# Three of the six tiles of a Fourier transform made from the other three by a product with a reversing permutation

## The chip, the cores and the metric

The kernel runs on 1 core of one Trainium2 chip. A core has TensorE (PE: matrix products; PEld is its weight load), VectorE (DVE), ScalarE (ACT), GpSimd (POOL) and SyncE (SP, which here issues all DMAs). The metric is the device time of one execution in microseconds, of which the profile's span covers all but 2 us. Lower is better.

## The reference

Three stages follow each other on 4 batches of 768 tokens. The first is an attention with a decaying state, in 8 heads of width 48; its result is x, [4, 768, 384]. The second mixes x by a Fourier transform and a normalised channel product, the third by a product over tokens and one over channels:

```python
def _moe_ref(x, w_ch1, w_ch2):
    X = np.fft.fft(x, axis=1)
    X = np.fft.fft(X, axis=2)
    mixed = np.real(X).astype(np.float32)
    u = x + mixed
    ...
    ch = np.maximum(un @ w_ch1, 0.0) @ w_ch2
    return (u + ch).astype(np.float32)

def _moe2_ref(x, w_tok1, w_tok2, w_ch1, w_ch2):
    xt = x.transpose(0, 2, 1)
    h = np.maximum(xt @ w_tok1, 0.0) @ w_tok2
    u = x + h.transpose(0, 2, 1)
    h2 = np.maximum(u @ w_ch1, 0.0) @ w_ch2
    return (u + h2).astype(np.float32)
```

## The kernel before

The attention runs in 24 chunks of 128 tokens, m = 0 to 23; b = m // 6 is the batch and j = m % 6 the chunk in it. In a chunk TensorE turns keys, makes the scores of chunk m and the output y of chunk m - 1 between them, updates the state, and turns y of chunk m - 1. ScalarE and VectorE do the elementwise work on gates, queries and keys for a part of three chunks, six chunks ahead, in steps that hang on each other: on ScalarE squares, magnitudes (Ln and Exp), inverses, factors, arctangents, sines; on VectorE logs (with a scan), tangents, phases (with a scan), products. Two loads of function tables fall into each part (L776 and L779). The last such part starts with m = 21, so from m = 20 on ScalarE has only copies.

The Fourier transform of batch b - 1 is done between the chunks of batch b. It is called a pass here: pass one is m = 6 to 11, pass two m = 12 to 17, pass three m = 18 to 23; the fourth batch is transformed after the attention. VectorE folds the sequence (fold_sequence), so that 384 rows stand for 768. At j=1 width_transform gives a_sb, cosine part and sine part of 193 columns each (FH = 193, since the other 191 columns mirror them). Then sequence_transform makes six tiles of 128 rows: for each one matmul with alt for the middle row, three with the cosine table cs and three with the sine table ss, all fp32, into the two halves of a bank of PSUM (f_bank, in turn). transformed_at says at which j: tile 0 at 2, tiles 1 and 2 at 3, tiles 3 and 4 at 4, tile 5 at 5. add_transform on VectorE adds a tile to y in four operations (cosines minus sines into the low columns, cosines plus sines mirrored into the high ones); added_at says when, one chunk later at the latest. SyncE stores the rows as u.

The order of the work is written out by hand, one program for each engine, with semaphores between them. An engine does its list strictly in order. In the profile's names h_area holds y_sb, cs and ss, res_area holds a_sb, cd and sd, bank is a bank of PSUM, late_area holds a_mid and small constants, tok_raw holds alt.

After the attention comes the channel product s0. TensorE does the width transforms, the transposes of the first normed batch (L243), six tiles of the sequence transform, then hidden (three fp32r matmuls for each of three k, L233 to L235, 12 tiles). From the third tile on, hidden waits until low_hidden (L209) on VectorE has freed the bank of the tile two before. Between its four-operation adds VectorE makes w2l (low_w2_sixth, L134, six parts) from w2h, which ScalarE has made in three copies (high_w2, L88). keep_busy (L1256) are matmuls of 384 columns whose result is not used, eight at each j=0.

## Time and profile before

| what | value |
|---|---|
| median of 3 runs | 1034.1 us (1032.19 to 1034.24) |
| the profiled execution | 1034.1 us, span 1032.1 us |
| TensorE busy | 971.1 us, 94% of the span |
| VectorE busy | 497.2 us, 48% |
| ScalarE busy | 360.7 us, 35% |
| attention and transforms | up to about 358 us of the span |
| the two channel stages | the rest |

Busy shares are means over all stages. For a stage one reads the timelines: which engine is idle, and what ended its idle time. A row of a timeline has the start, the time, the engine, the line, the operation, output<-input, the shape and, in brackets, how long the engine was idle before it and who released it. A matmul in fp32 leaves two records.

### The profile page before, as it was taken

Reading aid. Unit: us, or ns where it says so; the run is one execution under the profiler, and the core shown is the slowest. Engines: PE = TensorE matmul, PEld = TensorE weight load, DVE = VectorE, ACT = ScalarE, POOL = GpSimd, SP = SyncE. Lnnn points to the kernel's source line nnn. Section 1 sums busy time; section 2 is a strip of 40 time slices with the busy share of each in tenths; the row PEclk is TensorE's granted clock in tenths of the full one; section 3 lists DMA queues with packets and bytes.
Section 4 is the critical chain, followed back from the end, with each engine's and each line's share of the span. In section 5 each row is a group of like instructions: output and inputs, shape, how many; then the busy total and the mean of one; then the engine's idle time right before and its main releaser. Section 6 shows DMA issues by size and latency. Waiting matters only on the chain.

```text
span 1032.1 us, 15436 instructions
## 1 busy us (share of the span) xinstructions
PE 971.1 (94%) x6154; PEld 942.8 (91%) x6154; DVE 497.2 (48%) x798; ACT 360.7 (35%) x541; POOL 16.4 (2%) x12
## 2 busy tenths in 40 slices
PE   0389999999999999999999999999999999999997
PEld 0268799899898999999999999999999999999997
DVE  5887889989836825233243223442233214223220
ACT  7787777867412321122112122341212203121120
POOL 0000000000000000000000000040000000000000
PEclk9889999999999999999999999999999999999999
DMA  6689986996691191110110110010020001000000
GB/s 212 193 235 313 281 236 180 267 239 174 165 349 43 47 347 36 46 61 30 47 60 30 53 46 16 17 54 24 1 69 8 15 15 53 23 0 23 9 16 25
DMA packets 96741, 104.72 MB, mean 101 GB/s; under 512 B 13104, under 2 KB 90288, under 8 KB 96688
## 3 DMA queue, kind: packets, MB, share of 16 engines
q1 hardware_dynamic: 96688, 104.00, 34.4%
q8 instruction: 35, 0.57, 0.2%
q14 instruction: 18, 0.15, 0.0%
HBM read 70.86 MB, written 33.11 MB: 101 GB/s over the span
## 4 chain that ended last, share of the span: by engine, by line
PE 90%; ACT 4%; DVE 3%; issue 1%; DMA 1%; SPq 0%; DVEq 0%; ACTq 0%
PE bank L233 21%; PE bank L235 21%; PE bank L234 21%; PE score_banks L1167 5%; PE bank L1189 3%; PE bank L1187 3%; PE bank L1256 3%; PE bank L1232 3%; PE bank L1199 2%; PE bank L1250 2%; PE bank L1248 2%; PE score_banks L243 1%; PE bank L1159 1%; PE bank L1246 1%; ACT w_area L764 1%
## 5 line engine op out<-in xcount | busy, mean ns | idle before, releaser
L121 ACT ACTIVATE hh<-bank 128x384 fp32r<-128x384 f32 x192 | 94.5, 492 | 375.0 <-PE bank L235 375.0
L209 DVE SCALAR_TENSOR_TENSOR hl<-bank,hh 128x384 fp32r<-128x384 f32 x192 | 107.0, 558 | 195.6 <-ACT hh L121 195.6
L233 PE MATMUL bank<-w2h,hh 128*128 128x384 f32 x576 | 193.3, 336 | 0.0
L233 PE MATMUL bank<-nTh,w1h 128*128 128x384 f32 x576 | 193.0, 335 | 0.0
L235 PE MATMUL bank<-w2h,hl 128*128 128x384 f32 x576 | 192.5, 334 | 0.0
L234 PE MATMUL bank<-w2l,hh 128*128 128x384 f32 x576 | 192.5, 334 | 0.0
L235 PE MATMUL bank<-nTh,w1l 128*128 128x384 f32 x576 | 192.4, 334 | 0.0
L234 PE MATMUL bank<-nTl,w1h 128*128 128x384 f32 x576 | 192.4, 334 | 0.0
L233 PEld LDWEIGHTS bank<-nTh,w1h 128*128 128x128 f32 x576 | 108.1, 188 | 0.4 <-issue 0.2
L234 PEld LDWEIGHTS bank<-w2l,hh 128*128 128x128 f32 x576 | 108.2, 188 | 0.0
L234 PEld LDWEIGHTS bank<-nTl,w1h 128*128 128x128 f32 x576 | 108.1, 188 | 0.0
L233 PEld LDWEIGHTS bank<-w2h,hh 128*128 128x128 f32 x576 | 108.1, 188 | 0.0
L235 PEld LDWEIGHTS bank<-w2h,hl 128*128 128x128 f32 x576 | 108.1, 188 | 0.0
L235 PEld LDWEIGHTS bank<-nTh,w1l 128*128 128x128 f32 x576 | 108.1, 188 | 0.0
L1167 PE MATMUL score_banks<-w_area 96*128 96x128 f32 x384 | 74.1, 297 | 0.4 <-DMA w_area<-q_turn 0.4
L223 DVE TENSOR_TENSOR late_area<-bank,tok_raw 128x384 f32<-128x384 f32 x24 | 13.4, 558 | 125.1 <-PE bank L235 125.1
L1256 PE MATMUL bank<-late_area,ident 128*128 128x384 f32 x120 | 44.0, 518 | 28.7 <-DVE w_flat L958 28.7
L1189 PE MATMUL bank<-w_area 128*128 128x48 f32 (+1 forms) x384 | 66.7, 259 | 0.1
L1256 PEld LDWEIGHTS bank<-late_area,ident 128*128 128x128 f32 x120 | 23.5, 203 | 43.7 <-issue 31.7
L114 ACT ACTIVATE nTh<-score_banks 128x384 fp32r<-128x384 f32 x48 | 22.2, 491 | 113.5 <-PE score_banks L243 113.5
L1187 PE MATMUL bank<-late_area,w_area 96*128 96x96 f32 (+1 forms) x320 | 60.2, 270 | 0.0
L223 DVE TENSOR_TENSOR late_area<-bank,res_area 128x384 f32<-128x384 f32 x24 | 13.4, 558 | 92.7 <-PE bank L235 92.5
(159 smaller groups left out, 1311.5 us busy)
## 6 DMA issues: line engine op xcount, KB each, us to landing
w_area<-k_turn SPq DMA_DIRECT2D x24, 384.0 KB, 5.4
w_area<-q_turn SPq DMA_DIRECT2D x24, 384.0 KB, 6.4
q_turn<-w_raw SPq DMA_DIRECT2D x30, 192.0 KB, 2.9
k_turn<-n_area SPq DMA_DIRECT2D x24, 192.0 KB, 2.6
k_turn<-w_flat SPq DMA_DIRECT2D x24, 192.0 KB, 3.1
u_scratch<-h_area SPq DMA_DIRECT2D x24, 192.0 KB, 5.3
w_raw<-in_moe_w_ch SPq DMA_DIRECT2D x2, 2304.0 KB, 12.9
x_flat<-u_scratch SPq DMA_DIRECT2D x4, 1152.0 KB, 10.2
```

The lines of the kernel that those rows point to most:

```text
L114: self.nc.scalar.activation(self.nTh[:, :, i * P:(i + 1) * P], self.tr_bank[i % 2][:, 0:DM].rearrange("p (k t) -> p k t", k=KD), ACT.Copy) ...
L121: self.nc.scalar.activation(self.hh[:, m, :], self.mm_bank[(g * (KF + TPG) + m) % 2][:, 0:TG], ACT.Relu).then_inc(self.h_high, 1)
L209: self.nc.vector.scalar_tensor_tensor(out=self.hl[:, m, :], in0=self.mm_bank[(g * (KF + TPG) + m) % 2][:, 0:TG], scalar=0.0, in1=self.hh[: ...
L223: self.nc.vector.tensor_tensor(self.out_sb[:, i % 2, :], self.mm_bank[2 + t % 2][:, 0:DM], self.res[:, i, :], ALU.add).then_inc(self.out_r ...
L233: self.nc.tensor.matmul(out, lh, rh, start=(n == 0), stop=False)
L234: self.nc.tensor.matmul(out, lh, rl, start=False, stop=False)
L235: last = self.nc.tensor.matmul(out, ll, rh, start=False, stop=(n == len(pairs) - 1))
L1167: made = mm(sc_bank[h // 4][:, (h % 4) * P:(h % 4 + 1) * P], kT[:, r, h, :], qT[:, r, h, :], start=True, stop=True)
L1187: mm(y_bank[:, with_next(h)], qT[:, m % RING, h, :], state[:, n % 3, with_next(h)], start=True, stop=False)
L1189: made = mm(y_bank[:, own], pr[:, h, :], v_sb[:, p.s, m - p.first, own], start=not later, stop=True)
L1232: last = mm(f_bank[(m + 1) % 2][:, part * FH:(part + 1) * FH], fold[:, part, k_, m * P:(m + 1) * P], table[:, k_, :], start=(k_ == 0), sto ...
L1256: mm(f_bank[0][:, 0:S // 2], ident[:, :], blank[:, :], start=True, stop=True)
```

## The change

The transform of the sequence of real data is even in its cosine part and odd in its sine part. So rows 1 to 383 give rows 767 to 385 when cosines and sines are combined with the other sign. The kernel after makes tiles 0, 1 and 2 as before. ScalarE copies the cosine half to cos_part. VectorE makes cos - sin and cos + sin in pq and adds them to y. Row 384, the end row, is made by four matmuls with one output row (end_transform) and copied into pq (end_row). The other tiles, in the order 5, 4, 3, are one product of 386 columns each: the table flip, a permutation that reverses rows 1 to 127 and keeps row 0, times pq of tile 0, 1 or 2. Since row 0 of the mirrored tile belongs to the next one, ScalarE first moves rows: first_row_moved (row 0 of tile 1 to tile 0) and other_rows_moved (the first rows of the next tiles to tiles 1 and 2). VectorE adds such a tile in two operations. The tables cs and ss have 385 and 384 columns for 768.

The tiles stand at other chunks: 0 at j=2, 1 at j=3, 2 and the first reversed one at j=4, the other two at j=5. After the attention tiles 0 to 2 come ahead of the transposes 4 and 5, the reversed ones behind; VectorE adds tiles 0 to 2 before low_normed 4 and 5, and makes w2l behind the last three adds; ScalarE does its copies and row moves before high_normed 4 and 5 and high_w2.

```diff
+        HT = NT // 2
+        cs, ss = in_h(P, KD, S // 2 + 1), in_h(P, KD, S // 2)
+        pq, flip = in_h(P, HT + 1, 2 * FH), in_h(P, P)
+        cos_part = in_h(P, 2, FH)
+        in_h(P, 2 * KD * S - KD * (S + 1) - (HT + 2) * 2 * FH - P)
...
-            return {2: [0], 3: [1, 2], 4: [3, 4], 5: [5]}.get(j, [])
+            return {2: [0], 3: [1], 4: [2, 3], 5: [4, 5]}.get(j, [])
 
         def added_at(m):
             b, j = divmod(m, NCH)
             n = b - 2 if j == 0 else b - 1
-            return [(n, i) for i in {3: [0], 4: [1, 2], 5: [3, 4], 0: [5]}.get(j, []) if n >= 0]
+            return [(n, i) for i in {3: [0], 4: [1], 5: [2, 3], 0: [4, 5]}.get(j, []) if n >= 0]
+
+        def tile_of(i):
+            return i if i < HT else NT - 1 - (i - HT)
...
+            def end_row(b):
+                act.wait_ge(end_made, b + 1)
+                act.wait_ge(rows_moved, 2 * b)
+                A(pq[0:1, HT, :].rearrange("p (o n) -> p o n", o=2),
+                  f_bank[1][0:1, 0:FH].rearrange("p (o n) -> p o n", o=1).broadcast_to([1, 2, FH]),
+                  ACT.Copy).then_inc(end_ready, 1)
+
+            def cosines_copied(b, i):
+                act.wait_ge(b_made, b * NT + i + 1)
+                if b * HT + i >= 2:
+                    act.wait_ge(b_half, b * HT + i - 1)
+                A(cos_part[:, (b * HT + i) % 2, :], f_bank[i % 2][:, 0:FH], ACT.Copy).then_inc(cos_copied, 1)
+
+            def first_row_moved(b):
+                act.wait_ge(b_half, b * HT + 2)
+                act.wait_ge(b_added, b * NT + 1)
+                A(pq[0:1, 0, :], pq[0:1, 1, :], ACT.Copy).then_inc(rows_moved, 1)
+
+            def other_rows_moved(b):
+                act.wait_ge(b_added, b * NT + HT)
+                act.wait_ge(end_ready, b + 1)
+                act.wait_ge(rows_moved, 2 * b + 1)
+                A(pq[0:1, 1:HT, :], pq[0:1, 2:HT + 1, :], ACT.Copy).then_inc(rows_moved, 1)
...
+                if b and j == 2:
+                    end_row(b - 1)
+                if b:
+                    for n in transformed_at(j):
+                        if n < HT:
+                            cosines_copied(b - 1, n)
+                if b and j == 4:
+                    first_row_moved(b - 1)
+                if b and j == 5:
+                    other_rows_moved(b - 1)
...
+            end_row(B - 1)
+            for n in range(HT):
+                cosines_copied(B - 1, n)
+            first_row_moved(B - 1)
+            other_rows_moved(B - 1)
             s0.high_normed(act, 0, range(4, 6))
...
-                n = b * NT + i
-                x = y_sb[:, n % YR, :]
+                n, t = b * NT + i, tile_of(i)
+                x = y_sb[:, (b * NT + t) % YR, :]
+                low, high = x[:, 0:FH], x[:, DM - 1:FH - 1:-1]
+                one, two = f_bank[i % 2][:, 0:FH], f_bank[i % 2][:, FH:2 * FH]
                 dve.wait_ge(b_made, n + 1)
-                cc, sn = f_bank[i % 2][:, 0:FH], f_bank[i % 2][:, FH:2 * FH]
-                low, high = x[:, 0:FH], x[:, DM - 1:FH - 1:-1]
-                V.tensor_tensor(low, low, cc, ALU.add)
-                V.tensor_tensor(high, high, cc[:, 1:FH - 1], ALU.add).then_inc(b_half, 1)
-                dve.wait_ge(b_half, n + 1)
-                V.tensor_tensor(low, low, sn, ALU.subtract)
-                V.tensor_tensor(high, high, sn[:, 1:FH - 1], ALU.add).then_inc(b_added, 1)
+                if i < HT:
+                    less, more = pq[:, t, 0:FH], pq[:, t, FH:2 * FH]
+                    cos = cos_part[:, (b * HT + i) % 2, :]
+                    dve.wait_ge(cos_copied, b * HT + i + 1)
+                    V.tensor_tensor(less, cos, two, ALU.subtract)
+                    V.tensor_tensor(more, cos, two, ALU.add).then_inc(b_half, 1)
+                    dve.wait_ge(b_half, b * HT + i + 1)
+                    V.tensor_tensor(low, low, less, ALU.add)
+                    V.tensor_tensor(high, high, more[:, 1:FH - 1], ALU.add).then_inc(b_added, 1)
+                else:
+                    V.tensor_tensor(low, low, two, ALU.add)
+                    V.tensor_tensor(high, high, one[:, 1:FH - 1], ALU.add).then_inc(b_added, 1)
...
             s0.low_w1(dve, 2)
+            for i in range(HT):
+                add_transform(B - 1, i)
             s0.low_normed(dve, 0, 4)
             s0.low_normed(dve, 0, 5)
-            for i in range(NT):
+            for i in range(HT, NT):
                 add_transform(B - 1, i)
+                s0.low_w2_sixth(dve, i - HT)
...
+            def end_transform(b):
+                pe.wait_ge(a_ready, (b + 1) * KD)
+                last = S // 2
+                mm(f_bank[1][0:1, 0:FH], alt[:, 0:1], a_mid[:, :], start=True, stop=False)
+                for k_ in range(KD):
+                    made = mm(f_bank[1][0:1, 0:FH], cs[:, k_, last:last + 1], a_sb[:, k_, 0:FH],
+                              start=False, stop=(k_ == KD - 1))
+                made.then_inc(end_made, 1)
+
             def sequence_transform(b, m):
-                if m < 2:
-                    pe.wait_ge(a_ready, b * KD + 2 + m)
+                if m == 0:
+                    end_transform(b)
+                if m == 1:
+                    pe.wait_ge(end_ready, b + 1)
+                if m >= 2:
+                    pe.wait_ge(b_added, b * NT + m - 1)
+                out, t = f_bank[m % 2], tile_of(m)
+                if m < HT:
+                    rows = slice(t * P, (t + 1) * P)
+                    mm(out[:, 0:FH], alt, a_mid[:, :], start=True, stop=False)
+                    for k_ in range(KD):
+                        mm(out[:, 0:FH], cs[:, k_, rows], a_sb[:, k_, 0:FH], start=False, stop=(k_ == KD - 1))
+                    for k_ in range(KD):
+                        last = mm(out[:, FH:2 * FH], ss[:, k_, rows], a_sb[:, k_, FH:2 * FH],
+                                  start=(k_ == 0), stop=(k_ == KD - 1))
                 else:
-                    pe.wait_ge(b_added, b * NT + m - 1)
-                if m == 0:
-                    pe.wait_ge(a_ready, (b + 1) * KD)
-                rows = slice(m * P, (m + 1) * P)
-                out = f_bank[m % 2]
-                mm(out[:, 0:FH], alt, a_mid[:, :], start=True, stop=False)
-                for k_ in range(KD):
-                    mm(out[:, 0:FH], cs[:, k_, rows], a_sb[:, k_, 0:FH], start=False, stop=(k_ == KD - 1))
-                for k_ in range(KD):
-                    last = mm(out[:, FH:2 * FH], ss[:, k_, rows], a_sb[:, k_, FH:2 * FH],
-                              start=(k_ == 0), stop=(k_ == KD - 1))
+                    pe.wait_ge(rows_moved, 2 * b + min(m - HT + 1, 2))
+                    last = mm(out[:, 0:2 * FH], flip, pq[:, NT - 1 - t, :], start=True, stop=True)
                 last.then_inc(b_made, 1)
...
             width_transform(B - 1, 2)
+            for n in range(HT):
+                sequence_transform(B - 1, n)
             s0.transposes(pe, 0, 4)
             s0.transposes(pe, 0, 5)
-            for n in range(NT):
+            for n in range(HT, NT):
...
-    ws = 2 * np.pi * (np.arange(S // 2)[:, None] * np.arange(S)[None, :] % S) / S
+    ws = 2 * np.pi * (np.arange(S // 2)[:, None] * np.arange(S // 2 + 1)[None, :] % S) / S
     alt = np.where(t % 2 == 0, 1.0, -1.0) * (u == 0)
     wf = 2 * np.pi * (np.arange(DM)[:, None] * np.arange(DM)[None, :] % DM) / DM
     sf = 2 * np.pi * (np.arange(S)[:, None] * np.arange(S)[None, :] % S) / S
     named = dict(seq_cos=np.cos(sf), seq_sin=np.sin(sf), width_cos=np.cos(wf), width_nsin=-np.sin(wf),
-                 ident=ident, mask=mask, cd=np.cos(wd), sd=np.sin(wd), cs=np.cos(ws), ss=np.sin(ws), alt=alt)
+                 ident=ident, mask=mask, cd=np.cos(wd), sd=np.sin(wd), cs=np.cos(ws), ss=np.sin(ws[:, 0:S // 2]), alt=alt, flip=1.0 * (u == (P - t) % P))
```

The order on ScalarE at j=4 and j=5 of pass two, from the magnitudes of the next part to the turned y of chunk 16. First before (the step at L709 is the last of the magnitudes, L714 to L723 are inverses and factors, L757 copies y, L764 is the turned y):

```order
L709 ACTIVATE w_area<-n_area 128x1152 [waits vec_step_1,vec_step_0]
L757 ACTIVATE h_area<-bank 128x384 [waits u_stored_3,y_made]
L764 ACTIVATE w_area<-bank 128x3x128 [waits folded,tr_made]
L714 ACTIVATE n_area<-n_area 128x1152 [waits vec_step_0]
L716 ACTIVATE n_area<-n_area 128x1152 [waits act_step_0]
L721 ACTIVATE tok_raw<-x_flat 128x1152 [waits vec_step_0]
L723 ACTIVATE x_flat<-x_flat 128x1152 [waits act_step_0]
L757 ACTIVATE h_area<-bank 128x384 [waits u_stored_4,y_made]
L779 ACT_TABLE_LOAD
L764 ACTIVATE w_area<-bank 128x3x128 [waits folded,tr_made]
```

The same stretch after (L798 copies the cosines of tile 2, L803 is first_row_moved, L809 other_rows_moved; the other lines are those of before, moved down):

```order
L721 ACTIVATE w_area<-n_area 128x1152 [waits vec_step_1,vec_step_0]
L769 ACTIVATE h_area<-bank 128x384 [waits u_stored_3,y_made]
L798 ACTIVATE h_area<-bank 128x193 [waits b_half,b_made]
L803 ACTIVATE h_area<-h_area 1x386 [waits b_added,b_half]
L776 ACTIVATE w_area<-bank 128x3x128 [waits folded,tr_made]
L726 ACTIVATE n_area<-n_area 128x1152 [waits vec_step_0]
L728 ACTIVATE n_area<-n_area 128x1152 [waits act_step_0]
L733 ACTIVATE tok_raw<-x_flat 128x1152 [waits vec_step_0]
L735 ACTIVATE x_flat<-x_flat 128x1152 [waits act_step_0]
L769 ACTIVATE h_area<-bank 128x384 [waits u_stored_4,y_made]
L815 ACT_TABLE_LOAD
L809 ACTIVATE h_area<-h_area 1x772 [waits rows_moved,end_ready,b_added]
```

Two copies stand now between the copy of y and the turned y at j=4, and the move of the other rows stands behind the table load at j=5. TensorE's reversing products (L1327) wait for rows_moved.

The order on VectorE after the attention, from the add of tile 2 to the first low_hidden (L1061 to L1065 are an add in four operations, L1067 and L1068 one in two, L190 is low_normed, L134 makes w2l, L209 is low_hidden). Before, the last two adds:

```order
L1006 TENSOR_TENSOR h_area<-h_area,bank 128x193 [waits b_made]
L1007 TENSOR_TENSOR h_area<-h_area,bank 128x191
L1009 TENSOR_TENSOR h_area<-h_area,bank 128x193 [waits b_half]
L1010 TENSOR_TENSOR h_area<-h_area,bank 128x191
L134 TENSOR_TENSOR w2l<-w_flat,w2h 128x768 [waits w2_high_0]
L1006 TENSOR_TENSOR h_area<-h_area,bank 128x193 [waits b_made]
L1007 TENSOR_TENSOR h_area<-h_area,bank 128x191
L1009 TENSOR_TENSOR h_area<-h_area,bank 128x193 [waits b_half]
L1010 TENSOR_TENSOR h_area<-h_area,bank 128x191
L134 TENSOR_TENSOR w2l<-w_flat,w2h 128x768 [waits w2_high_0]
```

After:

```order
L1065 TENSOR_TENSOR h_area<-h_area 128x191
L190 TENSOR_TENSOR nTl<-score_banks,nTh 128x3x128 [waits nt_high_0] x2
L1067 TENSOR_TENSOR h_area<-h_area,bank 128x193 [waits b_made]
L1068 TENSOR_TENSOR h_area<-h_area,bank 128x191
L134 TENSOR_TENSOR w2l<-w_flat,w2h 128x768 [waits w2_high_0]
L1067 TENSOR_TENSOR h_area<-h_area,bank 128x193 [waits b_made]
L1068 TENSOR_TENSOR h_area<-h_area,bank 128x191
L134 TENSOR_TENSOR w2l<-w_flat,w2h 128x768 [waits w2_high_0]
L1067 TENSOR_TENSOR h_area<-h_area,bank 128x193 [waits b_made]
L1068 TENSOR_TENSOR h_area<-h_area,bank 128x191
L134 TENSOR_TENSOR w2l<-w_flat,w2h 128x768 [waits w2_high_0] x4
```

The six parts of w2l, one behind each of six adds before, stand now behind the last three adds, four of them in a row at the end, ahead of the first low_hidden. On ScalarE the copies of w2 stand behind the copies and row moves of the transform:

```order
L790 ACTIVATE h_area<-bank 1x386 [waits rows_moved,end_made]
L798 ACTIVATE h_area<-bank 128x193 [waits b_half,b_made] x3
L803 ACTIVATE h_area<-h_area 1x386 [waits b_added,b_half]
L809 ACTIVATE h_area<-h_area 1x772 [waits rows_moved,end_ready,b_added]
L114 ACTIVATE nTh<-score_banks 128x3x128 [waits tr_made_0] x2
L88 ACTIVATE w2h<-w_flat 128x1536 [waits w2_in]
L88 ACTIVATE w2h<-w_flat 128x1536 x2
```

There the first four rows are new.

## Rows read from the trace of the kernel before

**Rows 1.** The page: an engine's busy us, share of the span, instructions.
```profile
PE 971.1 (94%) x6154; PEld 942.8 (91%) x6154; DVE 497.2 (48%) x798; ACT 360.7 (35%) x541; POOL 16.4 (2%) x12
```

**Rows 2.** Busy time by engine (PE, PEld, DVE, ACT, POOL), clock, DMA; pass two.
```profile
194.40:265.00 70.60, 69.55 (x553) 65.81 (x553) 64.78 (x86) 50.22 (x62) 0.00 (x0) 1.00 0.86 220
```

**Rows 3.** TensorE's waits, 71 to 380 us: total, times, longest.
```profile
PE bank L1159 <- ACT w_area L764: 3.9, 15, 0.3
PE bank L1232 <- DVE w_area L998: 1.6, 1, 1.6
```

**Rows 4.** The chain of waits: start, us, what (two records a matmul).
```profile
254.54 0.98 PE bank L1248 x6
...
265.01 5.16 PE bank L1256 x16
...
275.75 1.07 PE bank L1217 x6
```

**Rows 5.** TensorE's timeline, pass two: start, us, line, tile, count.
```profile
246.06 0.49 PE L1246 MATMUL bank<-late_area,tok_raw 128*128 128x193 f32 x2
...
248.34 0.49 PE L1208 MATMUL bank<-ident,h_area 128*128 128x128 f32 x3
...
254.03 0.51 PE L1246 MATMUL bank<-late_area,tok_raw 128*128 128x193 f32 x2
```

**Rows 6.** ScalarE's timeline, pass two, j=3 to 5.
```profile
236.06 0.49 ACT L764 ACTIVATE w_area<-bank 128x384 f32<-128x384 f32 x1 [5.33 <-PE bank L1208]
...
240.57 1.28 ACT L776 ACT_TABLE_LOAD   x1
...
241.87 1.16 ACT L700 ACTIVATE x_flat<-x_flat 128x1152 f32<-128x1152 f32 x1
...
246.33 0.47 ACT L757 ACTIVATE h_area<-bank 128x384 f32<-128x384 f32 x1
...
251.65 1.17 ACT L721 ACTIVATE tok_raw<-x_flat 128x1152 f32<-128x1152 f32 x1
...
254.40 1.28 ACT L779 ACT_TABLE_LOAD   x1
```

**Rows 7.** VectorE's timeline, pass two: first product, scan.
```profile
239.83 1.36 DVE L957 TENSOR_TENSOR n_area<-w_flat,w_raw 128x1152 f32<-128x1152 f32 x1
...
249.05 2.56 DVE L904 TENSOR_TENSOR_SCAN x_flat<-x_flat,late_area 128x1152 f32<-128x1152 f32 x1
```

**Rows 8.** ScalarE and TensorE, pass three and after it, timelines.
```profile
324.11 0.49 ACT L757 ACTIVATE h_area<-bank 128x384 f32<-128x384 f32 x1 [4.13 <-PE bank L1189]
...
324.64 0.49 PE L1246 MATMUL bank<-late_area,tok_raw 128*128 128x193 f32 x2
...
334.60 0.30 ACT L769 ACTIVATE late_area<-bank 1x193 f32<-1x193 f32 x1
```

**Rows 9.** The fourth batch and first hidden tiles, timelines of three engines.
```profile
343.75 0.49 ACT L773 ACTIVATE res_area<-bank 128x386 f32<-128x386 f32 x1
...
344.88 4.24 ACT L88 ACTIVATE w2h<-w_flat 128x1536 fp32r<-128x1536 f32 x3
...
358.05 0.47 PE L233 MATMUL bank<-nTh,w1h 128*128 128x384 f32 x1
...
361.32 0.33 PE L233 MATMUL bank<-nTh,w1h 128*128 128x384 f32 x1
...
359.58 0.95 DVE L134 TENSOR_TENSOR w2l<-w_flat,w2h 128x768 fp32r<-128x768 f32 x1
...
360.48 0.56 DVE L209 SCALAR_TENSOR_TENSOR hl<-bank,hh 128x384 fp32r<-128x384 f32 x1
```

**Rows 10.** TensorE around its low clock; then busy time and clock.
```profile
335.37 3.75 PE L1232 MATMUL bank<-res_area,w_area 128*128 128x193 f32 x12 [1.59 <-DVE w_area L998]
...
336.00:337.00 1.00, 1.00 (x5) 1.00 (x4) 1.00 (x2) 0.27 (x1) 0.00 (x0) 0.50 0.00 0
```

20 lines of the change are left out of this document (13 added, 7 removed).

## The prediction

> **What bounds the kernel now.** I read the page first: the busy line gives TensorE 94% of the span [rows 1]. The reader is to see there that a matmul taken away is time taken away, if nothing else becomes late. Then the busy time of one stretch: the second of the three passes that transform a batch beside the attention of the next (m = 12 to 17), from 194.40 to 265.00 us, has TensorE busy 69.55 of 70.60 us, but VectorE 64.78 and ScalarE 50.22 too [rows 2]. Then the list of waits of TensorE: in all three passes its only repeated wait is 0.25 to 0.3 us behind a copy of ScalarE [rows 3]. So the passes run at TensorE's pace, and the other two engines are a few microseconds from being late. The question is therefore not only what the change takes from TensorE, but whom it makes TensorE wait for; for that I read the timelines of ScalarE and VectorE at the places where the new copies stand.
>
> **What TensorE loses and gains.** In the chain of waits six records, which are three 128x193 matmuls, take 0.98 us, so 0.327 us each; sixteen records, eight 128x384 matmuls, take 5.16 us, so 0.645 each [rows 4]. (The profile has two records for each fp32 matmul.) A tile of the sequence transform has 7 of the first kind, 2.28 us: tile 4 starts at 246.06 and its successor at 248.34 [rows 5]. Each pass loses three tiles, 6.85 us, and gains three products with the reversing table, 3 x 0.645 = 1.94, and the end row, four matmuls with one output row. Their price is that of their 193 columns, as the rows with one output row show (L1217, six records in 1.07 us, in the chain), so 1.31. Net 3.60 us a pass, 14.4 us in four: 1019.7 us if nothing waits. That is one end of what this can do.
>
> By place (j is the number of the chunk in its batch): j=2 costs 1.31; j=3 gives 2.28, so that its end is 0.97 early; j=4 gives 2.28 - 0.645 = 1.63 less a wait; j=5 has two reversing products, 1.29, where one tile stood, and gives 0.99 less a wait.
>
> **The wait at j=4, passes one and two.** The reversing product needs first_row_moved, which stands on ScalarE behind the magnitudes of the next part, the copy of y and the copy of the cosines. In pass two, before, ScalarE copied y at 246.33 [rows 6]. The chain to there starts with the copy at 236.06, released by TensorE, and has no gap, so it comes 0.97 early: 245.35. Then, one after another, the y copy (one of 0.49 us hands over after about 0.4), cosines 0.25 (L769, of the same 193 columns, lasts 0.30 [rows 8]) and the row move 0.49 (price of the copy with 386 columns, L773 [rows 9]): ready at 246.5. The first tile of this chunk was done at 246.06 before [rows 5], so tile 2 is done at 245.1. Wait 1.35; j=4 gives 0.28. The end of j=4 is then 1.25 early.
>
> **The wait at j=5, passes one and two.** other_rows_moved stands behind inverses, factors, the copy of y and, last, the load of a table (L779). Before, L721 began at 251.65, as soon as the scan of VectorE ended (249.05 + 2.56); that scan hangs on products, which began at 239.83 when ScalarE's sines were done, and these on TensorE's tile [rows 6, 7]. All of it comes 1.0 early and no more, so the table is loaded at 254.7 instead of 254.40 + 1.28 = 255.7 [rows 6]. The move of 772 numbers in one partition I take at 0.83, between the 0.49 of 386 columns and the 1.16 of 1152: ready at 255.5. TensorE is done with its scores at 254.03 - 1.2 = 252.85 [rows 5]. Wait 2.7; j=5 gives -1.7. Pass: -1.31 + 2.28 + 0.28 - 1.71 = **-0.46**, a loss, twice (pass one has the same instructions 70.6 us earlier): -0.9.
>
> The Trainium skill ("ScalarE: Activation LUTs", What ACT_TABLE_LOAD costs) says that a table load is followed by a drain, 2.66 us together. The trace shows a load at 240.57 and the next instruction at 241.87, with no drain behind it [rows 6]. By the rule the wait at j=5 would be 1.38 us longer in two passes, and the sum 2.8 us worse; I go by the trace.
>
> **Pass three** has no such chains: ScalarE waits for TensorE all the time (4.13 us ahead of the y copy at 324.11 [rows 8]). At j=4 the wait is the two copies alone, 0.07 + 0.25 + 0.49 + 0.06 = 0.85, so j=4 gives 0.78. At j=5 the y copy that starts at 324.11 hands over after 0.4, then 0.83 and 0.06: 0.7 us later than the scores' end at 324.64 [rows 8]; j=5 gives 0.29. Pass: -1.31 + 2.28 + 0.78 + 0.29 = **+2.04**.
>
> **The fourth batch**, between the attention and the channel product. I count in the time of before (all of it lies 1.1 us earlier by the passes' sum, which changes nothing in it). a_sb is whole at 343.75 + 0.49 [rows 9]. TensorE: end row and three tiles from 344.30 to 352.47, six transposes to 353.1, first reversing product at 353.3. VectorE adds tile 2 until 354.2 (four operations in about 1.2); ScalarE moves the rows until 355.05; second product 355.1 to 355.75. The third waits for tile 3 to be added, and VectorE has low_normed of tiles 4 and 5 ahead of that, which wait for ScalarE's copies behind the row move: 357.0 to 357.65. So TensorE is at the channel product 0.4 us early (358.05 before [rows 9]), and that is not what counts. Before, ScalarE's three copies of w2 (L88) ran from 344.88, 4.24 us, while TensorE had tiles to do [rows 9]. Now they stand behind the row move and two copies: 355.8 to 360.0. VectorE's six parts of w2l, 0.95 us each, filled its gaps between tiles; now they come behind add 3, one after each of the last three adds and then three more. They start when the first third of w2h is there, 357.2; six parts that hand over after some 0.92 (5.5) and two adds of two operations (1.2) end at 363.9, where the list was done at 360.48 before [rows 9]. Only then does low_hidden free a bank. The third hidden tile, begun at 361.32 before [rows 9], waits for the first: 363.9 + 0.56 + 0.06 = 364.5. **-3.2 us**. Bounds: no loss if the banks came free in time (+0.4), -3.2 as reckoned.
>
> **The clock.** In the fourth batch TensorE is idle 3.6 us ahead of that tile, and 1.2 + 1.3 us shortly before. In the trace an idle 1.59 us, with 0.46 us and one-row matmuls ahead of it, is followed by a granted clock of 0.50, its 1.2 GHz level [rows 10], and there the twelve records of L1232 take 3.75 us, where twelve such records at 2.4 GHz take 2 x 0.98 = 1.96 [rows 4]: 1.8 lost. I take one such fall: **-1.8**; the bounds are 0 and three falls (also one at each 2.7 us wait of j=5), -5.4. The Trainium skill ("TensorE: Matmul & The Clock Gate", What's actually happening) says that the low rate is the default and activity releases it; rows 10 agree.
>
> **Elsewhere.** VectorE loses six operations a pass, which covers nothing that TensorE waits for. The tables are 1.2 MB smaller, but TensorE waited for no table in a pass [rows 3]: nothing. Moved stores of u leave later by a chunk and are read much later.
>
> **Sum**: -0.9 + 2.0 - 3.2 - 1.8 = -3.9 us. The profiled execution took 1034.1 us (span 1032.1), which is the median: **1038.0 us**.
>
> **Rivals.**
> 1. No waits for rows: the rows come in time in all passes, only the fourth batch loses its 3.2: 1034.1 - 10.8 + 3.2 = 1026.5. The place is L1327 at j=5, and it decides whether other_rows_moved ends before TensorE's scores do, that is whether ScalarE comes to it 2.7 us earlier than I reckon. For it: ScalarE is busy only 50.22 of 70.60 us [rows 2]. Against it: its idle time lies elsewhere, and from the sines on its work is a chain [rows 6]. Half of the waits gone gives about 1031. Chance 0.2 for this side.
> 2. The waits as above without a new fall of the clock, 1036.2; or w2l late by half as much, 1034.6. For it: the idle stretches are broken by short work. 0.2, of which 0.15 inside the bound of no change.
> 3. Clock falls also at j=5, where TensorE idles 2.7 us at once, longer than the 1.59 of rows 10: place L1327, price 1.8 each, decided by whether the idle stretch exceeds what rows 10 show: 1041.6. 0.15.
> 4. VectorE becomes the bound of the passes: 64.78 of 70.60 busy, and it would bind only if a pass came down below about 64. That is under the full gain; no chance of its own.
> My forecast has 0.45.
>
> What a measurement of this kernel can tell from no change is about 0.2%, 2.1 us: faster is below 1032.0, slower above 1036.2. Faster 0.2; no change 0.15; slower 0.65 (0.45 + 0.15 + 0.05 of rival 2). The range 1029 to 1042 takes in rival 3, most of the half-way case of rival 1, and leaves out the full gain.
>
> **What the profile after would show.** Right: TensorE's waits name ScalarE's row moves, about 1.35 and 2.7 us in two passes, 0.85 and 0.7 in the third; a wait of some 3.6 us for L209 early in the channel product; w2l ending about 3.5 us later against hidden tile 0; a stretch at 0.5 clock there. Wrong: no wait at L1327, or one under 1 us at j=5, or the third hidden tile on time. The forecast falls if the passes get shorter by more than 2 us each.

## The result, and the profile after

The changed kernel takes 1045.64 us (median of 4 runs, 1040.90 to 1049.96), the kernel before in the same comparison 1033.14 (1031.52 to 1034.24): ratio 1.0124, 95% interval [1.0093, 1.0155]. It is slower, as forecast, but by 12.5 us where 3.9 were forecast, and outside the range. The four runs fall in two pairs: 1040.9 and 1041.5 us at a mean clock of 0.986 and 0.985, 1049.8 and 1050.0 at 0.976; the median lies between them, where no run is. The profiled execution is one of the second pair, with a span of 1047.8 us, 15.7 above that of before. Of all executions reported here one, of 1059.7 us in the repetition of this kernel (after_again), lies over 1.5% above the fastest of its kernel, counts as slow, and stands in no ratio.

The page first, the busy line (us, share, instructions) and TensorE's clock in 40 slices of the span; they answer to [rows 1]:

```profile
PE 971.2 (93%) x6042; PEld 933.0 (89%) x6042; DVE 489.3 (47%) x774; ACT 371.0 (35%) x565; POOL 16.4 (2%) x12
...
PEclk9789998898999999999999999999999999999999
```

TensorE has 112 instructions fewer and is busy for as long as before, 971.2 us against 971.1. The 14 us of matmuls are gone, so the rest must run more slowly: the second line has an 8 in the slices at about 170, 190 and 250 us. The windows of pass one (first row) and pass two, each from j=2 to the next j=2, answer to [rows 2]; then three single microseconds (columns: length, busy PE, PEld, DVE, ACT, POOL, clock, DMA share, GB/s):

```profile
142.15:220.89 78.74, 74.36 (x524) 67.48 (x524) 63.86 (x80) 54.80 (x71) 0.00 (x0) 0.89 0.80 213
220.89:297.28 76.39, 71.75 (x524) 65.67 (x524) 58.49 (x76) 47.13 (x64) 0.00 (x0) 0.93 0.65 174
170.00:171.00 1.00, 1.00 (x6) 1.00 (x7) 1.00 (x2) 1.00 (x1) 0.00 (x0) 0.50 0.00 0
190.00:191.00 1.00, 1.00 (x2) 0.43 (x2) 1.00 (x1) 0.00 (x0) 0.00 (x0) 0.50 0.92 252
247.00:248.00 1.00, 1.00 (x6) 1.00 (x6) 0.97 (x4) 0.98 (x3) 0.00 (x0) 0.50 0.03 8
```

The same stretches took 70.8 and 70.6 us before. Now pass one takes 78.7 and pass two 76.4, at mean clocks of 0.89 and 0.93, where [rows 2] had 1.00. In single microseconds the clock is 0.50, the 1.2 GHz level, from about 167 to 179 (10.2 us in all, by the sum over the windows), 188 to 196 (6.8), 246 to 257 (10.2) and 376 to 380 (3.4). Before, between the start and the last microseconds, there was one such stretch, 335 to 339. It is gone: the same wait for L1049, 1.58 us, now has no fall behind it, and its twelve records last 2.24 us, not 3.75 [rows 10].

What low clock costs among the attention's products, TensorE's timeline in pass one, low and high (start, us, line, tile, count):

```profile
170.54 0.58 PE L1250 MATMUL bank<-late_area,w_area 96*128 96x96 f32 x2
170.91 0.55 PE L1252 MATMUL bank<-w_area 128*128 128x48 f32 x2
171.26 0.76 PE L1230 MATMUL score_banks<-w_area 96*128 96x128 f32 x2
...
184.65 0.36 PE L1250 MATMUL bank<-late_area,w_area 96*128 96x96 f32 x2
184.85 0.35 PE L1252 MATMUL bank<-w_area 128*128 128x48 f32 x2
185.03 0.45 PE L1230 MATMUL score_banks<-w_area 96*128 96x128 f32 x2
185.32 0.36 PE L1250 MATMUL bank<-late_area,w_area 96*128 96x96 f32 x2
```

Such a group of three takes 0.67 us (184.65 to 185.32) at 2.4 GHz and 1.28 (170.54 to 171.82, the next) at 1.2.

TensorE's waits, 60 to 400 us (total, times, longest), for [rows 3]:

```profile
PE bank L1327 <- ACT h_area L809: 6.3, 4, 2.3
PE bank L1222 <- ACT w_area L776: 3.6, 14, 0.3
PE bank L1327 <- ACT h_area L803: 3.0, 4, 0.9
PE bank L233 <- DVE hl L209: 3.0, 1, 3.0
PE bank L1295 <- DVE w_area L1049: 1.6, 1, 1.6
PE bank L1327 <- DVE h_area L1068: 1.0, 1, 1.0
PE bank L1250 <- DVE w_area L1036: 0.6, 2, 0.3
```

They name what the prediction named: the row moves L803 and L809 in all passes, and L209 ahead of the third hidden tile. (The next in the list are of 0.6 us and less, once each.) Where they stand, TensorE's timeline in pass one, pass two, and the fourth batch:

```profile
165.59 0.46 PE L1250 MATMUL bank<-late_area,w_area 96*128 96x96 f32 x2 [0.32 <-DVE w_area L1036]
...
180.69 0.89 PE L1327 MATMUL bank<-h_area 128*128 128x386 f32 x2 [0.92 <-ACT h_area L803]
...
189.62 2.91 PE L1327 MATMUL bank<-h_area 128*128 128x386 f32 x4 [2.35 <-ACT h_area L809]
...
268.35 1.54 PE L1327 MATMUL bank<-h_area 128*128 128x386 f32 x4 [2.35 <-ACT h_area L809]
...
368.46 0.64 PE L233 MATMUL bank<-nTh,w1h 128*128 128x384 f32 x1
...
375.02 0.44 PE L233 MATMUL bank<-nTh,w1h 128*128 128x384 f32 x1 [2.97 <-DVE hl L209]
```

Set beside the low stretches, the waits do not pair off with them. The stretch from 188 begins inside the 2.35 us wait of pass one, and that from 376 about 1 us behind the wait for L209. But those of 10.2 us, from 168 and 246, begin at j=4, some 2 us behind the waits of 0.32 and 0.33 us for L1036 (165.59, and 244.34 in pass two) and about 12 us ahead of the first wait for a row move; and behind the 2.35 us wait of pass two, 268.35, there is no fall.

ScalarE and VectorE in pass two answer to [rows 6, 7]: the table load, the row move behind it, the scan, and a wait of the phases, 2.41 us where before had 0.89, that was not reckoned with:

```profile
266.07 1.28 ACT L815 ACT_TABLE_LOAD   x1
267.36 0.85 ACT L809 ACTIVATE h_area<-h_area 1x772 f32<-1x772 f32 x1
...
236.68 1.36 DVE L985 SCALAR_TENSOR_TENSOR n_area<-n_area,w_raw 128x1152 f32<-128x1152 f32 x1 [2.41 <-ACT w_area L746]
...
257.23 2.56 DVE L955 TENSOR_TENSOR_SCAN x_flat<-x_flat,late_area 128x1152 f32<-128x1152 f32 x1
```

The fourth batch on ScalarE and VectorE answers to [rows 9]:

```profile
366.65 4.22 ACT L88 ACTIVATE w2h<-w_flat 128x1536 fp32r<-128x1536 f32 x3
...
370.95 3.55 DVE L134 TENSOR_TENSOR w2l<-w_flat,w2h 128x768 fp32r<-128x768 f32 x4
374.42 1.01 DVE L209 SCALAR_TENSOR_TENSOR hl<-bank,hh 128x384 fp32r<-128x384 f32 x2
```

### The profile page after: what moved, and what is told of

Same layout as the page of the kernel before. It is cut to its first block, busy times and chain, and to the rows that moved or that the text cites. A ratio compares the mean times of both kernels' runs of the same rounds, so it can differ in the third digit from the quotient of the medians.

```text
span 1047.8 us, 15252 instructions
## 1 busy us (share of the span) xinstructions
PE 971.2 (93%) x6042; PEld 933.0 (89%) x6042; DVE 489.3 (47%) x774; ACT 371.0 (35%) x565; POOL 16.4 (2%) x12
## 4 chain that ended last, share of the span: by engine, by line
PE 85%; ACT 7%; DVE 5%; issue 2%; DMA 0%; SPq 0%; DVEq 0%; ACTq 0%
PE bank L233 21%; PE bank L235 21%; PE bank L234 21%; PE score_banks L1230 4%; PE bank L1252 3%; PE bank L1332 3%; PE bank L1250 3%; PE bank L1295 2%; PE bank L1262 2%; PE score_banks L243 1%; DVE n_area L990 1%; PE bank L1321 1%; PE bank L1323 1%; PE bank L1222 1%; PE bank L1327 1%
## 5 line engine op out<-in xcount | busy, mean ns | idle before, releaser
L209 DVE SCALAR_TENSOR_TENSOR hl<-bank,hh 128x384 fp32r<-128x384 f32 x192 | 106.9, 557 | 197.2 <-ACT hh L121 197.2
L1230 PE MATMUL score_banks<-w_area 96*128 96x128 f32 x384 | 77.7, 309 | 0.4 <-DMA w_area<-q_turn 0.4
L1250 PE MATMUL bank<-late_area,w_area 96*128 96x96 f32 (+1 forms) x320 | 62.3, 277 | 0.6 <-DVE w_area L1036 0.6
L1252 PEld LDWEIGHTS bank<-w_area 128*128 128x128 f32 x384 | 59.7, 198 | 0.1
```

The lines of the kernel that those rows point to most:

```text
L209: self.nc.vector.scalar_tensor_tensor(out=self.hl[:, m, :], in0=self.mm_bank[(g * (KF + TPG) + m) % 2][:, 0:TG], scalar=0.0, in1=self.hh[: ...
L1230: made = mm(sc_bank[h // 4][:, (h % 4) * P:(h % 4 + 1) * P], kT[:, r, h, :], qT[:, r, h, :], start=True, stop=True)
L1250: mm(y_bank[:, with_next(h)], qT[:, m % RING, h, :], state[:, n % 3, with_next(h)], start=True, stop=False)
L1252: made = mm(y_bank[:, own], pr[:, h, :], v_sb[:, p.s, m - p.first, own], start=not later, stop=True)
```

## The experiments

Executions of one kernel differ by up to 13.9 us here (after_busy3), with the one of 1059.7 us by 17.6, together with their mean clock: over the five of the repetition below, a mean clock lower by 0.001 goes with 1.06 us, which that one execution all but sets; the two pairs of after give 0.9. So the table gives the product of time and mean clock too, about the time with the half-speed stretches counted at full speed. It hardly scatters: 1020 to 1023 for before, whose own mean clock is 0.989 (the start of the span, alike in all, has the most of that). The ratios are against the runs of before that were timed together with the kernel (medians 1032.8 to 1033.6). The product flatters a kernel whose waits lie in low stretches, since a slowed TensorE waits less.

| kernel | median (range, runs) us | ratio to before, 95% interval | mean clock, median | time x clock |
|---|---|---|---|---|
| before | 1032.8 (1032.1 to 1034.9, 24) | 1 | 0.989 | 1021.7 |
| after | 1045.6 (1040.9 to 1050.0, 4) | 1.0124 [1.0093, 1.0155] | 0.981 | 1025.3 |
| after_again | 1042.3 (1042.1 to 1059.7, 5) | 1.0094 [1.0080, 1.0109] | 0.982 | 1024.7 |
| before_moved | 1035.1 (1033.6 to 1037.9, 10) | 1.0019 [1.0010, 1.0029] | 0.990 | 1023.9 |
| after_busy3 | 1053.2 (1046.2 to 1060.1, 4) | 1.0169 [1.0131, 1.0207] | 0.976 | 1028.7 |
| after_still | 1039.2 (1035.0 to 1044.0, 8) | 1.0058 [1.0038, 1.0078] | 0.980 | 1018.5 |
| after_tail | 1039.4 (1038.3 to 1046.5, 5) | 1.0058 [1.0041, 1.0075] | 0.982 | 1021.8 |
| before_wait | 1039.3 (1036.5 to 1041.2, 6) | 1.0061 [1.0048, 1.0075] | 0.986 | 1025.1 |
| after_fill | 1042.2 (1040.9 to 1043.1, 4) | 1.0089 [1.0074, 1.0103] | 0.987 | 1028.6 |
| end_row_later | 1046.5 (1037.4 to 1047.0, 4) | 1.0100 [1.0065, 1.0135] | 0.976 | 1022.1 |
| busy_first | 1044.8 (1043.5 to 1049.2, 4) | 1.0107 [1.0092, 1.0121] | 0.984 | 1028.1 |
| early_rows | 1039.7 (1039.2 to 1041.5, 4) | 1.0064 [1.0049, 1.0078] | 0.977 | 1015.8 |
| early_fill | 1043.9 (1035.1 to 1044.9, 5) | 1.0109 [1.0095, 1.0124] | 0.974 | 1016.8 |
| early_fill_tail | 1032.8 (1030.1 to 1039.6, 12) | 1.0002 [0.9987, 1.0017] | 0.985 | 1016.8 |
| dense_behind | 1040.1 (1035.3 to 1045.4, 5) | 1.0069 [1.0042, 1.0095] | 0.984 | 1022.9 |
| fill_third | 1032.5 (1029.4 to 1041.4, 10) | 1.0011 [0.9985, 1.0037] | 0.986 | 1017.7 |
| mask_first | 1033.3 (1026.8 to 1034.3, 12) | 0.9990 [0.9975, 1.0005] | 0.984 | 1016.4 |
| turned_first | 1028.7 (1028.1 to 1031.0, 5) | 0.9962 [0.9948, 0.9975] | 0.988 | 1016.8 |
| **all_filled** | **1026.1 (1025.9 to 1027.1, 5)** | **0.9930 [0.9916, 0.9944]** | 0.989 | 1015.6 |

My theory was that waits of the reckoned kind explain a few us and that falls of the clock beside them explain the rest. The rivals were that the tiles' new places, or the thinness of TensorE's work at j=3, bring the falls without any wait.

**The kernel before with the tiles at the new chunks** (before_moved).

```diff
-            return {2: [0], 3: [1, 2], 4: [3, 4], 5: [5]}.get(j, [])
+            return {2: [0], 3: [1], 4: [2, 3], 5: [4, 5]}.get(j, [])
```

> The kernel before, all six tiles made as before, but at the places of the changed kernel: one at j=2, one at j=3, two at j=4, two at j=5. The work of TensorE is the same. Theory A (in the changed kernel the clock falls in the chunk after j=3 because only one dense tile stands there, so that the thin attention work comes sooner): granted clock 0.5 for some 10 us in one or two passes, time 1038 to 1045. Theory B (it falls because of the new waits): VectorE is not late here, no wait over 0.3 us, no fall in the passes, 1033 to 1035.

It costs 2.0 us by the ratio, and its profiled execution has before's clock and no fall in a pass, though the 0.32 us wait for VectorE of the kernel after stands in it too (and in pass two at 236.33):

```profile
164.72 0.46 PE L1189 MATMUL bank<-late_area,w_area 96*128 96x96 f32 x2 [0.32 <-DVE w_area L986]
```

So the places do not bring the 12.5 us. That they bring no falls at all is not shown: three of the ten executions have a mean clock of 0.985 to 0.987, where the lowest of before's 17 is 0.987, and the slowest took 1037.9 us.

**Unused matmuls at j=3** (after_busy3), behind the tile:

```diff
+                if b and j == 3:
+                    pe.wait_ge(b_added, (b - 1) * NT + 1)
+                    keep_busy(4)
```

> The changed kernel with four matmuls of 384 columns, whose result is not used, behind the tile at j=3 (2.58 us a pass, about what the moved tile took). Theory A: the falls in the chunk after j=3 are gone; 4.4 us saved in two passes against 2.6 us spent in three, so near the changed kernel's lower runs, 1040 to 1044, and its runs no longer lie 9 us apart. Theory B: VectorE is no longer late at j=4, since TensorE comes 2.6 us later, so the 0.33 us wait goes and the falls too: the same. If the falls stay, both are wrong.

1053.2 us, where both theories had 1040 to 1044: both are wrong by the words of the forecast. That no fall begins at j=3 or early in j=4 any more is as hoped, but longer ones begin at j=5: 20.4 us from 186 and 17.1 from 271, at the waits of 2.54 us for L809. Work filled in away from those waits left them in place, and falls with them.

**Without the waits for rows** (after_still): the reversing product reads fixed data in place of pq, so the mirrored tiles are not computed.

```diff
-                    pe.wait_ge(rows_moved, 2 * b + min(m - HT + 1, 2))
-                    last = mm(out[:, 0:2 * FH], flip, pq[:, NT - 1 - t, :], start=True, stop=True)
+                    last = mm(out[:, 0:2 * FH], flip, h_area[:, 0:2 * FH], start=True, stop=True)
```

> The changed kernel, but the three reversing products read a part of a table that nobody writes, and so wait for no moved rows; the mirrored tiles get wrong numbers. The waits at L1327 in the passes (0.92 + 2.35 us, twice, and 0.92 + 0.66) and 0.26 + 0.98 us in the fourth batch are gone: 8.1 us less wait. Theory B (waits cause the falls): the falls at j=5 go, and those after j=3 stay, since they come before it: 1033 to 1039. If the passes are bound by VectorE or ScalarE instead, a good part of the 8.1 us comes back as waits at L1250 or L1222.

1039.2 us, 6.4 below after and 3.1 below its repetition, at the upper end of the forecast, because another wait takes the place: at j=5 for tile 2 to be added, 1.88 us twice (the third, 0.51, is in the fourth batch).

```profile
PE bank L1326 <- DVE h_area L1065: 4.3, 3, 1.9
```

Falls of 3.4 us come with these two, from 184 and 256. The falls after j=3, which the forecast had as staying, are not in this trace.

**Only the order after the attention** (after_tail): high_w2 between the cosine copies, a part of w2l behind each add.

```diff
-            for n in range(HT):
-                cosines_copied(B - 1, n)
+            cosines_copied(B - 1, 0)
+            act.wait_ge(w2_in, 16)
+            s0.high_w2(act, 0)
+            cosines_copied(B - 1, 1)
+            s0.high_w2(act, 1)
+            cosines_copied(B - 1, 2)
...
             for i in range(HT):
                 add_transform(B - 1, i)
+                s0.low_w2_sixth(dve, i)
```

> The changed kernel with another order after the attention: ScalarE makes the first two thirds of w2h between the copies of cosines, VectorE makes a part of w2l behind each add. Forecast's step on w2l: the third hidden tile waited 2.97 us for VectorE; here VectorE's list ends some 2.5 us earlier, the wait is below 0.6 us, and the low clock that follows (2.0 us) goes with it: 4 to 5 us less than the changed kernel. If that wait costs nothing: no difference.

The wait for L209 is gone; time x clock falls by 3.5 against after, 2.9 against its repetition. The term w2l is confirmed in place and size. The low stretch near it does not go with it, as the forecast had it: one of 3.4 us stands there still, from 369. In passes one and two the same wait of 3.42 us for L809 has 20.5 us of low clock with it, from 185, and 3.4, from 267.

**The kernel before with only the wait** (before_wait): in passes one and two TensorE waits at j=5 until ScalarE has loaded the table.

```diff
+                if b in (1, 2) and j == 5:
+                    pe.wait_ge(tables_loaded, b)
```

> The kernel before with one thing added: in passes one and two TensorE waits at j=5, ahead of its tile, for ScalarE's load of the table (about 255.75 in pass two, so an idle 1.7 us, twice, 3.4 us in all), and ScalarE makes a copy of two numbers there. Theory A (what the changed kernel loses beyond its waits is the clock, which falls at such a wait and does not come back while the thin attention work lasts): a fall in some runs, 0.5 for 10 to 20 us each, time 1036 to 1050 with runs far apart. Theory B (a wait costs its length, a fall at most 1.8 us as forecast): 1036 to 1038, runs close together.

The waits in the profile, and the clock behind the first of them:

```profile
PE bank L1250 <- issue: 3.6, 2, 1.8
...
188.00:189.00 1.00, 1.00 (x5) 0.91 (x4) 1.00 (x1) 0.00 (x0) 0.00 (x0) 0.50 0.98 254
```

3.6 us of waiting cost 6.5 us at the median. The fall behind the first wait lasts 3.4 us, 186.3 to 189.7; behind the second there is none. Three of the six executions have a mean clock of 0.985, below every one of before in the comparison (0.988 to 0.990). Nothing of the change is in this kernel but the waits and a ScalarE copy of two numbers (0.20 us), so a wait at this place can bring a fall by itself. The falls of 10 to 20 us that theory A named did not come in the profiled execution.

**The wait filled with unused work** (after_fill): four matmuls of 384 columns ahead of the two reversing products.

```diff
+                if b and j == 5:
+                    fill(m, 4)
```

> The changed kernel with four matmuls of 384 columns without use (2.6 us) at j=5, ahead of the reversing products, in a bank that is free there; they stand where TensorE was idle 2.35 us. Theory A: no fall at j=5, some 7 to 10 us less than the changed kernel in its slow executions, runs closer together, 1036 to 1042. Theory B: the same time or up to 1 us more, since the wait was as long anyway.

No fall in a pass, and the schedule can be read undisturbed. The median is 3.5 us below after's and level with its repetition's: the unused work of 2.59 us in pass three, where the wait was 0.66, costs time too. Its timeline in pass two:

```profile
214.22 0.50 PE L1222 MATMUL bank<-ident,w_area 96*128 96x96 f32 x4
...
238.46 0.46 PE L1250 MATMUL bank<-late_area,w_area 96*128 96x96 f32 x2 [0.32 <-DVE w_area L1036]
248.68 0.89 PE L1327 MATMUL bank<-h_area 128*128 128x386 f32 x2 [0.92 <-ACT h_area L803]
258.67 1.54 PE L1327 MATMUL bank<-h_area 128*128 128x386 f32 x4 [0.83 <-ACT h_area L809]
...
286.80 0.50 PE L1222 MATMUL bank<-ident,w_area 96*128 96x96 f32 x4
```

The pass lasts 72.58 us against 70.61 before (212.48 to 283.09 at the same row): +1.97, and pass one +1.77. At j=5 the real wait is 2.59 (what the fill covers) + 0.83 = 3.42. In after it reads 2.35 only, since the slowed TensorE came late itself; and 3.42 is what the next run reads. The 0.32 us wait (238.46), behind which after had its fall, stands here with none.

**The same kernel again** (after_again).

> The changed kernel once more, for another trace of it. Theory A: low clock in another number of places, or of other lengths, than the first trace (0.5 from 167 to 179, 188 to 196, 246 to 257 and 376 to 380 us), waits of the same length, and the time follows the low clock: half of its length. Theory B: time lies in the waits, so the same trace with the same time.

Its profiled execution, 1059.7 us, has the long falls: 20.5 us from 185 and 20.5 from 267, both from inside the wait of 3.42 us; behind the 0.33 us waits at j=4 it has none. Its wait, the clock late in the stretch, and the unused matmuls at which the clock is back:

```profile
186.20 2.91 PE L1327 MATMUL bank<-h_area 128*128 128x386 f32 x4 [3.42 <-ACT h_area L809]
...
204.47 5.82 PE L1332 MATMUL bank<-late_area,ident 128*128 128x384 f32 x16
...
195.00:196.00 1.00, 1.00 (x6) 1.00 (x7) 0.96 (x2) 1.00 (x2) 0.00 (x0) 0.50 1.66 90
204.00:205.00 1.00, 1.00 (x5) 0.81 (x4) 0.60 (x2) 0.29 (x1) 0.00 (x0) 0.50 1.08 387
206.00:207.00 1.00, 1.00 (x5) 0.60 (x4) 1.00 (x2) 1.00 (x2) 0.00 (x0) 1.00 0.67 250
```

TensorE is busy 1.00 of such a microsecond, with attention products of 48 to 128 columns, and stays at 0.50 for 20 us. One such fall costs up to 10 us, as an estimate: half its length, less what it takes off later waits. That it lasts so long is not peculiar to this execution: after_tail has one of 20.5 us in one of 1046.5, and end_row_later one of 17.1.

**The end row later** (end_row_later): end_transform and end_row stand behind the turned y at j=2.

```diff
-                if m == 0:
-                    end_transform(b)
+                if b and j == 2:
+                    end_transform(b - 1)
```

> The changed kernel with one edit in the passes: the end row is made behind the turned y at j=2 instead of ahead of tile 0. If the 3.42 us wait at j=5 (forecast 2.7, since I let VectorE's products come 1.0 us early) is longer because the end row holds up y_turned, ScalarE's sines and VectorE's phases: VectorE's wait for L746 falls from 2.40 to about 1, no 0.32 us wait at L1250, and the wait at j=5 falls to 2.2 to 2.5 us. If not: they stay. Time 1037 to 1042, by the clock.

```profile
184.45 1.68 PE L1327 MATMUL bank<-h_area 128*128 128x386 f32 x4 [2.54 <-ACT h_area L809]
```

VectorE's wait of 2.40 us for the sines falls to 0.88, which is what before has there (0.89), the 0.32 at L1250 are gone, the wait at j=5 is 2.54 and that at j=4 1.36: the two numbers of the forecast (2.7 and 1.35) come back. So the end row at j=2, ahead of the turned y, was what made ScalarE late. The clock took back what that gave: 1046.5 us at 0.976, with falls of 17.1 us from 186 and 3.4 from 264, while one of the four took 1037.4 at 0.987.

**The eight unused matmuls moved** from the end of j=0 to the end of j=5 (busy_first).

```diff
+                if b in (1, 2) and j == 5:
+                    fill(m, 8)
-                if b and j == 0:
+                if b == 1 and j == 0:
```

> The changed kernel with the eight unused matmuls of 384 columns (5.2 us) of the end of j=0 moved to the end of j=5, right behind the late reversing products, in passes one and two; the number of matmuls is the same. Theory A (a fall at j=5 stays until dense work comes): falls at j=5 end after some 4 to 8 us instead of 20; execution times 1038 to 1044 and none near 1050 to 1060. Theory B (a fall has a fixed length): no difference from the changed kernel.

No fall near j=5 in its profile, but those at j=4 stay (10.2 us twice), and without the matmuls at j=0 a new wait of 1.6 us for ScalarE appears at L1295. Not conclusive.

**Rows ready early** (early_rows): tile 2 again at j=3, the end row as in end_row_later, first_row_moved before the table load of j=4, other_rows_moved in j=4, and after_tail's order at the end.

```diff
-            return {2: [0], 3: [1], 4: [2, 3], 5: [4, 5]}.get(j, [])
+            return {2: [0], 3: [1, 2], 4: [3], 5: [4, 5]}.get(j, [])
...
+                if b and j == 4:
+                    other_rows_moved(b - 1)
-                if b and j == 5:
-                    other_rows_moved(b - 1)
```

> Where the experiments point to: the changed kernel with tile 2 back at j=3, the end row behind the turned y at j=2 (so that ScalarE's sines do not come later), first_row_moved at j=4 ahead of the table load, other_rows_moved at j=4 behind the copy of y, and the order after the attention as in the run before. Reckoned: no wait for rows in the passes, masked just in time, 3.3 us gained in each of three passes, about 1 us after them: 1022 to 1026 if the clock stays up; if thin work alone lets the clock fall (four fifths of a pass without a dense tile), falls at j=4 or j=5 and 1030 to 1045.

No wait for rows is left in the passes, but with two dense tiles fewer at j=4 TensorE arrives at the turned y 2.67 us before ScalarE has copied y (L769), twice, and falls of 13.7 us follow, from 179 and 254:

```profile
177.46 0.55 PE L1272 MATMUL bank<-ident,h_area 128*128 128x128 f32 x3 [2.67 <-ACT h_area L769]
```

The lowest time x clock so far, 1015.8: the gain is there and the clock eats it.

**That wait filled** (early_fill): keep_busy(4) ahead of the turned y at j=4 in passes one and two. **And the end of the attention tidied too** (early_fill_tail): transposes 4 and 5 ahead of the end row, w2h and w2l between the tiles.

```diff
+                if b in (1, 2) and j == 4:
+                    pe.wait_ge(b_added, (b - 1) * NT + HT)
+                    keep_busy(4)
```

> The run with early rows, and in passes one and two four matmuls of 384 columns without use (2.6 us) at j=4, ahead of the turned y, where TensorE was idle 2.67 us for ScalarE's copy of y. Theory A (the falls of the clock follow the idle stretches and stay while work is thin; time is what the trace shows less half of the low length): no falls at 178 and 253, some 10 us less than with early rows alone, 1027 to 1031, below the kernel before. Theory B (the falls come from thin work, whatever the idle time): falls elsewhere, 1036 to 1042.

> The same, with another order after the attention: transposes 4 and 5 ahead of the end row, as in the kernel before, ScalarE's copies of w2 one each behind the normed copies, the end row and the first copy of cosines, w2l one part behind each add, first_row_moved ahead of the third copy of cosines. Expected 1 to 2 us less than the run with early rows and filler: the waits ahead of L1303 (0.58) and of the first reversing product (0.26) go, that ahead of the second becomes some 2 us instead of 0.98, and the third has none of its 0.97.

The first takes 1035.1 us in its profiled execution (mean clock 0.983), and 1040.5 to 1044.9 at 0.973 to 0.977 in the others, where 1027 to 1031 was expected: filling the wait in its own place did not keep the clock up in four of five. The second is level with before. It has the same passes as the first and, at the median, the same time x clock; that it takes 11 us less goes with the clock (0.985 against 0.974), and why the clock is higher is not shown. Its profiled execution has no fall in passes one and two, and one of 13.6 us from 327, behind the only long wait left there:

```profile
324.39 0.46 PE L1248 MATMUL bank<-late_area,w_area 96*128 96x96 f32 x2 [1.36 <-DVE w_area L1038]
...
330.00:331.00 1.00, 1.00 (x6) 0.68 (x4) 0.00 (x0) 0.00 (x0) 0.00 (x0) 0.50 0.00 0
```

The second half of this stretch, from 331 on, is no attention: waits of 0.46 and 0.64 us stand there, and the width products of 193 columns, whose first twelve records take 4.23 us. So not all of a long fall lies among thin attention products.

**That wait treated in three ways**: removed by VectorE's order (mask_first), filled with two unused matmuls (fill_third), left with eight behind it (dense_behind).

```diff
+                masked(m)
                 if m == NM - 1:
                     s0.normalised(dve, 0)
-                masked(m)
```

> On top of early_fill_tail VectorE makes the mask product of the last chunk (L1038) before the six operations that normalise the first batch (L178, 2.42 us in a row), so that TensorE does not wait 1.36 us for it in pass three. In the profile of early_fill_tail a low clock of 13.6 us (327 to 341) followed that wait. Theory P (a fall that comes amid thin attention products costs half of its 10 to 20 us, and the wait brings it on): the wait and the fall both go, -1.4 and about -6.8 us against a run that had the fall, so about 1026 us in the profiled run and a median of 1026 to 1028 against 1032.8, ratio 0.994 to 0.996. Rival F (falls come whether or not TensorE waited just before): only the 1.4 us goes, about 1031.4, ratio 0.999, and a low stretch of 10 us or more is still there near 327.

> On top of early_fill_tail two unused matmuls of 384 columns (2 x 0.645 = 1.29 us) stand before the outputs of the last chunk, where TensorE waited 1.36 us in pass three. The schedule is that of early_fill_tail. Theory P: the idle time is below 0.2 us there, no fall between 322 and 341, about 6.8 us less than a run that had it: 1025 to 1028, ratio 0.993 to 0.996. Rival F: unchanged, 1032.8, ratio 1.000, and the low stretch is still there.

> On top of early_fill_tail the wait of 1.36 us in pass three stays, and eight unused matmuls of 384 columns (5.16 us at 2.4 GHz) stand right behind it, ahead of the thin outputs of the last chunk. Theory D (what follows the wait sets how long the clock stays low; dense work ends it, thin work does not): a fall of 3.4 us at the most, or none; the 5.16 us of added work against up to 6.8 us saved: 1031 to 1033 in the profiled run. Rival L (a fall lasts 10 to 20 us whatever follows): the low stretch is still 10 us or longer, the added matmuls run at half speed for part of it, and the kernel takes 1037 to 1041.

In all three profiles the stretch from 327 is gone (mask_first has none after the start; fill_third has two of 3.4 us, near 332 and 353, dense_behind one, near 356). In dense_behind the wait of 1.41 us is still there:

```profile
324.19 5.40 PE L1380 MATMUL bank<-late_area,ident 128*128 128x384 f32 x16 [1.41 <-issue]
...
326.00:327.00 1.00, 1.00 (x5) 0.60 (x4) 0.00 (x0) 0.00 (x0) 0.00 (x0) 1.00 0.61 217
330.00:331.00 1.00, 1.00 (x11) 1.00 (x11) 0.00 (x0) 0.00 (x0) 0.00 (x0) 1.00 0.00 0
```

That agrees with theory D as to the low stretch, but the profiled time is 1035.4 where it had 1031 to 1033, the median of 1040.1 lies in rival L's 1037 to 1041, and three of the five runs had a mean clock of 0.978 to 0.984, and so fell somewhere. The ratios of the other two, 0.999 and 1.001, are rival F's (0.999 and 1.000), though the stretch that it wanted near 327 is not in their traces: five of the 12 executions of mask_first took 1026.8 to 1030.3 us, seven 1032.7 to 1034.3, at a clock of 0.981 to 0.984; of the ten of fill_third three took 1038.1 to 1041.4 at 0.977 to 0.980. Only one execution of a kernel has a trace; the other falls had to be found by another experiment.

**The last waits in the passes.** In mask_first two of over 0.3 us were left, 0.93 us each at the keys of chunks 12 and 18, for the turned y behind a table load. all_filled puts two of the eight unused matmuls there; turned_first makes the turned y before the load.

```diff
+                if m in (2 * NCH, 3 * NCH):
+                    pe.wait_ge(st_free, b * (NCH - 1))
+                    for _ in range(2):
+                        mm(st_bank[:, 0:S // 2], ident[:, :], blank[:, :], start=True, stop=True)
...
-                    keep_busy(8)
+                    keep_busy(8 if b == 1 else 6)
```

> On top of mask_first two of the eight unused matmuls of j=0 stand now ahead of the turned keys of chunks 12 and 18, where TensorE waited 0.93 us for ScalarE's turned y behind a table load; six stay at j=0. The undisturbed schedule becomes 1.9 us shorter. Of mask_first, 5 of 12 executions had a mean clock of 0.987 to 0.990 and took 1026.8 to 1030.3 us, the other 7 one of 0.981 to 0.984 and 1032.7 to 1034.3. Theory P: the falls of those 7 hang on the two remaining waits of 0.93 us amid thin work; with them gone nearly all executions are at 0.988 or above, median 1025 to 1027, ratio 0.993. Rival F: falls come in about half of the executions whatever the waits; the median stays at 1030 to 1032, ratio 0.997 to 1.000.

> On top of mask_first ScalarE makes the turned y of j=5 in passes one and two before it loads the table, not behind it. TensorE's wait of 0.93 us (L1220) goes, twice; ScalarE's chain of arctangents and sines starts 0.9 us later. Theory P: if no wait takes its place, as all_filled, 1025 to 1028. Rival S (the chain is then late): VectorE's phases and products start 0.9 us later, and a wait of 0.5 to 0.9 us appears at j=4 or j=5 of the next pass; 1031 to 1034, with the clock falls of mask_first.

all_filled: every execution at 0.988 to 0.990, 1025.9 to 1027.1 us, ratio 0.993 [0.992, 0.994], 7.5 us below before. It does the reference's whole computation and is the fastest kernel here. Theory P's figures are hit, rival F's (1030 to 1032) are missed; with five executions that is strong, not certain. turned_first takes the 0.93 us away too, gets a wait of 0.9 for the copy of y in exchange, and is at 0.986 to 0.990. That before had no falls in its passes fits too: its longest wait there is 0.3 us [rows 3]. The page's busy line and clock of all_filled:

```profile
PE 961.5 (94%) x6058; PEld 922.7 (90%) x6058; DVE 489.5 (48%) x774; ACT 370.5 (36%) x565; POOL 16.4 (2%) x12
...
PEclk9889999999999999999999999999999999999999
```

## Why the prediction was wrong

**The direction came out for its reason, not by luck.** All the waits that it named are there, and without the clock they and the new products alone make the kernel 5.7 us slower (below). Their order of size was not quite as given: undisturbed, the wait at j=5 (3.42) is the longest, not that for L209 (2.97).

**The step that failed is the clock**: "I take one such fall: -1.8", with rival 3's 1.8 for each further one. The count was wrong, since the profiled execution has three falls in the passes beside one in the hidden tiles, and the price more so. It was read from [rows 10], one fall of 3.4 us among the dense width products. Among the attention products at j=4 and j=5 the clock stayed low for 6.8 to 10.2 us in after, 20.5 in its repetition and in after_tail: 3.4 to 10 us lost each, as an estimate by half the length. In the profiled execution passes one and two are 7.9 and 5.8 us longer than before, of which the undisturbed schedule explains 1.77 and 1.97: the clock has 10.0, and 5.7 + 10.0 is the 15.7 by which the span grew. At the median the forecast's 1.8 stand against 6.8, namely 12.5 less 5.7; since that median lies between two pairs, the figure is soft (by after_again, 9.5 us above before, it is 3.8). The prediction's premise that activity gives the high clock back ([rows 10]) does not hold here as it stands: TensorE was busy 1.00 of each microsecond from 168 to 178 at a clock of 0.50. Nor was [rows 10] certain in itself: the same wait of 1.6 us has a fall at it in before, after_again and after_fill, and none in after.

Where the falls come was half right. Rival 3 had them at the waits of j=5, and some are there; but the two longest of the profiled execution stand ahead of all waits for rows, behind 0.32 us waits that after_again, after_fill, after_tail and before_moved have in the same place without a fall. What set those two off is not shown.

**The schedule was mis-sized by 3.6 us**: forecast +2.1 without the clock, measured 1.77 + 1.97 - 1.34 + 3.3 = +5.7 (passes one and two from after_fill; pass three from after, 297.28 to 347.42 against 283.89 to 335.37 of before; the last from after_fill, 339.43 to 368.71 against 335.37 to 361.32). By terms:

- Products, j=2 +1.31: it is 1.5 (a chunk of 12.04 us against 10.52). j=3, 2.28 early: exact. A reversing product hands over after 0.69 to 0.73, where 0.645 was taken.
- j=4, a wait of 1.35: it is 0.92 + 0.32. j=5, 2.7: it is 3.42. Both were reckoned from ScalarE's chain coming 0.97 to 1.0 early. The end row ahead of the turned y at j=2 holds up ScalarE's sines, and VectorE then waits 2.4 us for them; end_row_later brings back 1.36 and 2.54. Each step that is moved delays those behind it in the same chunk, and that one I had not followed.
- The row move, 0.83: 0.85. The table load: 1.28, with the next instruction 1.29 behind its start, so no drain here either, as the trace of before had it and not as the Trainium skill ("ScalarE: Activation LUTs", What ACT_TABLE_LOAD costs) says.
- Pass three, +2.04: +1.34. Its two waits, reckoned at 0.85 and 0.7, are 0.92 and 0.66; the terms of the first add up to 0.87 (and those of j=4 in the other passes to 1.40, not 1.35), which changes nothing. Fourth batch, -3.2, wait 3.6: -3.3, wait 2.97; after_tail shows the cause: with the parts of w2l spread over the adds the wait is gone.

**The rivals.** 1 (rows in time) did not happen, and early_rows shows why it could not without more: then the copy of y is late by 2.67. 2 (no new fall) did not happen either; even the fastest run of after, 1040.9, is above its 1036.2. 3 (falls at j=5) named the right kind of place and a fraction of the price. 4 played no part in after; in after_still the next wait is one for VectorE. The 0.65 for slower fits the result, which one result cannot prove; the range was too narrow above, because rival 3 had no bound on how long a fall lasts.

What stays open: what sets off the falls that stand behind no wait of over 0.33 us, why a fall behind the same wait lasts 3.4 us once and 20.5 another time (after_tail has both in one execution), in what share of executions a given wait brings one, and why early_fill and early_fill_tail differ.

## What to carry to other kernels

A wait of a microsecond or more amid small matmuls is not priced by its length: here it could bring 3.4 to 20.5 us of half speed, and no single one told which. Before work is taken out of such a stretch, the engines beside it must have their results early enough, or the hole is filled with unused matmuls in the very place of the wait; four unused matmuls elsewhere (after_busy3) did not help. One hole filled is not enough either: of the changed kernels only all_filled, where no wait of over 0.4 us is left in the passes, has before's clock in every execution. And judge such a change by several executions with their mean clocks, since time x clock shows a gain (in early_fill_tail 1016.8 against 1021.7) that the median hides.

## What was not expected of the hardware

- TensorE stays at 0.50 while it is busy 1.00 of each microsecond, for up to 20.5 us, most of them attention products of 48 to 128 columns; behind the same wait before the same work it is back after 3.4 us in pass two of after_tail.
- 3.6 us of waits in an otherwise unchanged kernel cost 6.5 us.
- Executions of one and the same kernel (after_busy3) lie 13.9 us apart, 1046.2 at a mean clock of 0.987 and 1060.1 at 0.970; in all_filled the five lie within 1.3.
